# Slots for 404 instead of 416 tokens per expert in a fused attention, mixture-of-experts and feed-forward kernel

## What is computed

```python
noisy = x @ w_gate + log1p(exp(x @ w_noise)) * noise
top2  = the two largest of the 8 columns, with softmax weights
out[t] = sum over its two experts e of weight * (max(x[t] @ w1[e], 0) @ w2[e])     # w1: 512x1024, w2: 1024x512
```

## Time and profile before

| | us |
|---|---|
| median of 3 runs | 729.0 (728.29 to 731.8) |
| the profiled execution, as timed | 732.01 |
| its span from first to last instruction | 730.2 |
| TensorE busy | 713.0 (98% of the span) |
| VectorE busy | 325.2 (45%) |
| ScalarE busy | 308.7 (42%) |
| GpSimd busy | 53.1 (7%) |

### The profile page before, as it was taken

One profiled execution on the slowest core, in us unless ns is written; L12 is line 12 of the kernel. 1 busy time (PEld: TensorE's weight loads), 2 busy tenths in 40 slices (PEclk: granted clock), 3 DMA queues, 4 the chain that ended last, 5 costly groups with the idle time before them and its releaser, 6 DMA issues.

```text
span 730.2 us, 10935 instructions
## 1 busy us (share of the span) xinstructions
PE 713.0 (98%) x4006; PEld 633.2 (87%) x4006; DVE 325.2 (45%) x855; ACT 308.7 (42%) x626; POOL 53.1 (7%) x68
## 2 busy tenths in 40 slices
PE   8999997999999999999999999999999999999997
PEld 4888897999999999999999997888887888878886
DVE  4776786534434353443434344655533233232221
ACT  3676782435444444445444432543433222232222
POOL 0000354000000000000000004111001110000000
PEclk9999999799999999999999999999999999999999
DMA  9987344475353414335353105554002110010001
GB/s 366 422 333 272 139 160 148 163 234 206 116 208 113 172 59 182 121 116 207 115 208 111 50 1 158 153 171 144 1 2 81 49 44 0 15 44 0 1 0 58
DMA packets 42546, 93.93 MB, mean 129 GB/s; under 512 B 3080, under 2 KB 11656, under 8 KB 42120
## 3 DMA queue, kind: packets, MB, share of 16 engines
q1 hardware_dynamic: 34824, 73.98, 28.6%
q0 software_dynamic: 3840, 12.59, 5.2%
q10 hardware_dynamic: 3840, 6.82, 2.5%
HBM read 70.30 MB, written 23.07 MB: 128 GB/s over the span
## 4 chain that ended last, share of the span: by engine, by line
PE 93%; DVE 2%; ACT 2%; issue 1%; DMA 1%; SPq 0%; POOL 0%; POOLq 0%; DVEq 0%; ACTq 0%
PE bank L1350 26%; PE bank L1352 25%; PE bank L1351 25%; PE bank L1284 2%; PE bank L1469 2%; PE bank L1511 2%; PE bank L1251 2%; PE bank L1281 2%; PE bank L1327 1%; PE bank L1387 1%; PE bank L1262 1%; PE bank L1534 1%; PE bank L1312 1%; PE bank L1264 1%; PE bank L1296 1%
## 5 line engine op out<-in xcount | busy, mean ns | idle before, releaser
L1350 PE MATMUL bank<-xh,w1h 128*128 128x416 f32 (+1 forms) x288 | 98.7, 343 | 0.8 <-issue 0.3
L1352 PE MATMUL bank<-xh,w1l 128*128 128x416 f32 (+1 forms) x288 | 98.0, 340 | 0.0
L1351 PE MATMUL bank<-xl,w1h 128*128 128x416 f32 (+1 forms) x288 | 97.3, 338 | 0.0
L1218 DVE SCALAR_TENSOR_TENSOR g<-bank,rel 128x512 f32<-128x512 f32 x48 | 33.2, 691 | 125.5 <-ACT rel L774 125.5
L774 ACT ACTIVATE rel<-bank 128x512 f32<-128x512 f32 x48 | 28.7, 598 | 136.6 <-PE bank L1352 136.6
L1350 PE MATMUL bank<-hh,w2h 128*128 128x416 f32 x224 | 79.3, 354 | 0.0
L1352 PE MATMUL bank<-hh,w2l 128*128 128x416 f32 x224 | 79.0, 353 | 0.0
L1351 PE MATMUL bank<-hl,w2h 128*128 128x416 f32 x224 | 78.2, 349 | 0.0
L1350 PE MATMUL bank<-zh,wih 128*128 128x512 f32 (+1 forms) x200 | 76.5, 382 | 0.1
L1350 PE MATMUL bank<-woh,gh 128*128 128x512 f32 x192 | 75.4, 393 | 1.0 <-ACT ost L770 1.0
L1352 PE MATMUL bank<-zh,wil 128*128 128x512 f32 (+1 forms) x200 | 76.1, 381 | 0.0
(11 more groups left out here) (145 smaller groups left out, 1253.1 us busy)
## 6 DMA issues: line engine op xcount, KB each, us to landing
w1r<-in_w SPq DMA_DIRECT2D x8, 2048.0 KB, 8.0
w2r<-in_w SPq DMA_DIRECT2D x7, 2048.0 KB, 9.2
x_by_slot<-zero SPq DMA_DIRECT2D x8, 832.0 KB
y_by_slot<-yst ACTq DMA_DIRECT2D x24, 256.0 KB, 6.2
qk_sb<-in_qk SPq DMA_DIRECT2D x3, 1920.0 KB, 20.8
xg<-x_by_slot SPq DMA_DIRECT2D x7, 768.0 KB, 7.6
win_raw<-in_w_in SPq DMA_DIRECT2D x16, 256.0 KB, 3.4
wout_raw<-in_w_out SPq DMA_DIRECT2D x16, 256.0 KB, 3.2
```

The lines of the kernel that those rows point to most:

```text
L1218: V.scalar_tensor_tensor(g[:, i % 2, :], bank[i % 2][:], 0.0, rel[:, i % 2, :], ALU.max, ALU.mult).then_inc(sq_done, 1)
L1350: MM(out_, wh, mh, start=start, stop=False)
L1351: MM(out_, wh, ml, start=False, stop=False)
L1352: return MM(out_, wl, mh, start=False, stop=stop)
```

## The change

CAP becomes 404. With it HALF becomes 202, LAST_ROWS 20, the second tile of each half 74 rows, and ZP 101: `zero_slots` sends 101 partitions instead of 104. The zero store of the second round is written with ZP in place of P partitions, and the last tile's copy of the last expert starts at a multiple of 32 partitions, as it did before (rows 96 to 127, of which the last 20 are stored).

```diff
-CAP = 416
+CAP = 404
...
             with sp.If(count > CAP):
-                sp.dma_start(ys[SLOTS:ROUNDS * SLOTS, :].rearrange("(n p) d -> p n d", p=P),
-                             zero[:].unsqueeze(1).to_broadcast([P, (ROUNDS - 1) * SLOTS // P, D])).then_inc(zero_y_st, 16)
+                sp.dma_start(ys[SLOTS:ROUNDS * SLOTS, :].rearrange("(n p) d -> p n d", p=ZP),
+                             zero[0:ZP].unsqueeze(1).to_broadcast([ZP, (ROUNDS - 1) * SLOTS // ZP, D])).then_inc(zero_y_st, 16)
...
                 rows = slice(0, P) if m < MT - 1 else slice(P - LAST_ROWS, P)
+                copied = slice(rows.start // BLOCK * BLOCK, P)
...
-                nc.scalar.copy(yst[rows, m, :], bank[LAST_YBANKS[m]][rows, :]).then_inc(y_sb, 1)
+                nc.scalar.copy(yst[copied, m, :], bank[LAST_YBANKS[m]][copied, :]).then_inc(y_sb, 1)
```

## The result

| | before | after |
|---|---|---|
| median of the runs | 730.3 us (728.29 to 731.8) | 959.43 us (958.56 to 963.85) |
| span of the profiled execution | 730.2 us | 957.5 us |
| TensorE busy | 713.0 us (98%) | 708.4 us (74%) |

The changed kernel takes 1.315 times as long (95% interval 1.311 to 1.319). The forecast was 967 us, in a range of 935 to 1000.

What follows compares the result with a forecast made beforehand. TensorE, busy for 98% of the span, was taken to bound the kernel. 732.0 - 6.7 (matmuls) + 235.2 (zero stores) + 5.2 (74-row loads) + 4.4 (clock) = 970.1 us profiled, 967 us against the 729.0 median; range 935 to 1000.

Steps and rivals of the forecast that it cites:

- the step on the zero stores: Zero stores of 101 partitions, a prime count, go on one DMA engine instead of 13; loads behind them wait.
- Its price: Zeros on one engine end at 302 us, w1r lands at about 309 instead of 73.8: a shift of 235.2 us.
- The signs: Profile after: DMA share 0.06, SP's zero stores issuing about 275 us, ACT idle until about 309, 2866 packets under 512 B.
- Who waits: ACT waits for w1r in step 14, TensorE within one attention step; POOL's wait for the zeros ends earlier, at about 304.
- The fourth rival: One engine, but w1r holds up neither ACT nor TensorE; POOL's late scatters delay expert 0's rows: 952 us, chance 0.05.
- The matmuls: 1344 matmuls lose 12 columns each, saving 5.0 ns apiece: 6.7 us; expert 0's halves, 208 to 202 columns, save 0.
- The step that told column-bound from load-bound: Weight loads can follow after 0.11 us, so columns pace the 416-column matmuls; the 208-column ones are bound by something else.
- The 74-row loads: Second tile of each half of expert 0 loads on 2 engines: twice 2.6, so 5.2 us, between 0 and 6.
- The clock: After TensorE's long pause, some 8.8 us at half clock cost 4.4 us; at least 0, up to 25.
- The sum: 732.0 - 6.7 + 235.2 + 5.2 + 4.4 = 970.1 us for the profiled execution; 967 us against the 729.0 median.
- The rule of the Trainium skill: For SP and ACT DMAs, engines used are the largest number up to 16 dividing both sides' slowest dimension; 101 gives one.

Runs made afterwards that it cites:

- the kernel with both DMA effects taken away: The 404-slot kernel with zeros on all 16 engines and 74-row loads split in 64 and 10 rows: 731.62 us against 738.96, again 724.95 against 731.76.

## Why the prediction was right, point by point

- **The cause** was the step on the zero stores, and it held: one engine, shown by the packet count (2866 forecast, 2866 counted), by the share of 0.07, by 103 partitions that do the same to 416 slots, and by zeros on 16 engines that undo it at 404.
- **Its price** was 235.2 us and measured 229.5. The term that was too large is the engine's rate: 25.1 GB/s, from 13 engines together, against 25.6 from one alone. 3232 packets of 79.9 ns are 258 us and not 264. The 103-partition kernel, forecast with the measured rate, came to 309.34 us where 309 was written.
- **The signs** held but for one: SP was to be busy with the zero stores for 275 us and was for 238 (18.50 to 256.84 us). The last store had left SP's hands 42 us before POOL went on at 298.72.
- **Who waits** held: ACT first, at the cast of w1r, and TensorE behind it. The fourth rival described the second wait behind it, and the run with w1r on the other queue put its time at 951 to 957 for a forecast of 952.
- **The matmuls**: 6.7 us forecast. The 144 matmuls of expert 1's hidden layer start every 184.2 ns (402.65 to 428.99 us), and every 189.6 before (167.86 to 194.97): 5.4 less, where 5.0 was taken. The experts' stage is 6.8 shorter, and the kernel with both DMA effects taken away is 6.8 below the kernel before, by the medians. That stage holds 1248 of the 1344 matmuls and also the smaller transposes, so of 5.5 ns for each matmul (6.8 / 1248) a small part isn't the matmuls' own. (The profiled execution of that kernel is the fastest of its six and 8.8 us below that of the 416-slot kernel with 16-engine zeros. Some 2 us of this are the clock's: after the pause for the second half's rows it was 0.50 until 132 us in the one and past 136 in the other. Why is open.) The step that told column-bound from load-bound was needed: the halves' matmuls with 202 columns still start every 0.11 us, as with 208.
- **The 74-row loads**: 5.2 us forecast, 4.1 measured with 416 slots and 4.7 with 404. The first place was taken too large, a wait of 1.5 to 1.8 us and not 2.6, and the second too small, 3.0 to 3.2 us more than the wait of 4.4 to 4.5 that stood there; together 4.5 to 5.0. From the issue to the transposes it is 5.8 to 6.1 us at the first place, where it was 4.1 without a wait, and 7.3 to 7.5 at the second, where it was 4.2. Why the same load takes longer at the second place is not shown.
- **The clock**: 4.4 us forecast. After the stall TensorE was granted 0.50 of full speed, the 1.2 GHz level, for some 8 us, as forecast; but it did attention steps then. The whole stretch from the cast to the first half's transposes grew by 3.5 us, and 1.7 of these are the wait for the 74 rows, which leaves 1.8. The 103-partition kernel has the same stall without 74-row loads: its stretch grew by 1.7 (309.34 to 342.66, against 73.82 to 105.41), and its whole span by 236.0 where its cast is 235.5 later. So the clock cost under 2 us. That ACT and DVE partly pace these steps would explain it, and is not shown.

```profile
304.00:308.00 4.00, 2.16 (x10) 2.16 (x11) 1.59 (x8) 3.94 (x13) 1.44 (x1) 0.50 0.38 149
308.00:312.00 4.00, 4.00 (x20) 3.67 (x21) 2.88 (x17) 1.37 (x5) 0.82 (x1) 0.50 0.05 20
312.00:316.00 4.00, 4.00 (x32) 3.56 (x30) 2.43 (x24) 2.90 (x8) 0.15 (x1) 0.79 0.18 68
316.00:320.00 4.00, 4.00 (x38) 3.61 (x37) 2.19 (x10) 2.64 (x7) 0.00 (x0) 1.00 0.03 6
```

- **The sum** forecast a profiled execution of 970.1 us and it was 959.29, 10.8 less: 5.7 from the engine's rate, 2.6 from the clock, 0.8 from the 74 rows (1.7 and 2.7 in the table), and 1.7 from the matmuls' 0.1 and two stretches that the sum had at nothing, the one before expert 1 (0.9, some 0.5 of it expert 0's 96 output matmuls) and the last layer (0.7). The cost at half clock was taken from a stretch in which TensorE was busy throughout and ACT and DVE for under a third; no run shows 4.4 us after the long pause.
- **The rule of the Trainium skill** ("DMA: Bandwidth & Descriptors", section "Why a DMA increments its semaphore by 16 and not by 1") holds in every transfer counted here: 104, 101, 103, 68, 119, 74, 20, 15, 10, 6 and 4 rows. The packets under 512 B of every run come out by it exactly, as 16 for each DMA and 128 for the noise load, less what the stores and loads on fewer engines lack: 3016 for 103 partitions, 3018 and 3162 for 68 and 119, 2976 for 74 rows and 6, 2938 for 64 and 10. So does its statement on order within one queue (section "Queues, rings and completion order"), as far as the run with w1r on ACT's queue tells: there w1r was in within 11.65 us of its issue, and in the changed kernel, behind the zeros, it landed after them.

## What to carry to other kernels

When a size changes, factor what becomes the outermost dimension of every DMA: 104 to 101 partitions is 3% fewer bytes and 1 engine instead of 13. Split such a transfer in multiples of 16 and a rest; one more issue is cheap beside it (64 and 10 rows instead of 74 gave back 4.7 us). A store that nobody waits for yet still holds back what is behind it in its queue, and the count of small packets on the page tells, without any experiment, how many engines all the DMAs use together.

## What the runs showed of the hardware that I had not expected

- One DMA engine that carries a stream of 2 KB packets alone is hardly faster than one of 13 (25.6 against 25.1 GB/s) or one of 16 (407 / 16 = 25.4): idle neighbours give it next to nothing.
- A short pause can bring the clock down as well as a long one. In the first profile of the 404-slot kernel with 16-engine zeros all engines but POOL stood still for some 3 us up to 117 us, and the trace names no engine of the core that they waited for; the granted clock then fell to 0.50. From the first set of transposes to the second this execution took 32.9 us; the one profiled the second time, without that pause, took 26.7. Nothing was tried on where that pause comes from. The kernel with zeros on 7 engines has one like it, 3.5 us before 124.33, and all four profiles from that chip need 36 to 38 us from the cast to the first transposes, where the trace of the kernel before has 31.6, so it says nothing on the 74 rows. (Windows of the first profile, columns as above.)

```profile
115.00:120.00 5.00, 2.23 (x17) 2.26 (x18) 2.48 (x13) 2.66 (x6) 0.61 (x1) 0.93 0.25 95
120.00:125.00 5.00, 5.00 (x25) 5.00 (x26) 1.93 (x9) 1.10 (x2) 1.95 (x2) 0.50 0.14 52
```

- The wait for the 74 rows can do the same, and doesn't always. In the second profile of that kernel TensorE stood still for 1.53 us before the first transposes at 106.94, and the granted clock was 0.50 for some 3 us from 107.4; this and the longer second wait make the 26.7 us, where the kernel with 64 and 10 rows takes 22.6. After waits of 1.81 us (416 slots, 74-row loads) and 1.70 us (the changed kernel) at the same place the clock stayed at 1.00. What decides is open. (Windows of the second profile.)

```profile
106.00:110.00 4.00, 3.06 (x19) 3.06 (x19) 1.38 (x8) 1.13 (x6) 2.92 (x3) 0.68 0.56 209
110.00:114.00 4.00, 4.00 (x34) 4.00 (x34) 2.30 (x13) 2.22 (x6) 0.98 (x1) 0.89 0.36 138
```
